# Attention of the first batch in token-tile order, with its feed-forward begun after 256 tokens

## The reference, cut to what matters

```python
scores = scale * q @ k.T + bias          # [B=4, H=8, S=576, S], masked to 0 <= i-j < 128
x = softmax(scores) @ v                  # -> [2304, 512]
x = relu(x @ w_in) ** 2 @ w_out          # 512 -> 2048 -> 512
out = sum_e P[:, e:e+1] * (relu(x @ w1[e]) @ w2[e])   # P: gate, 8 rounds of row and column scaling
```

## Time and profile before

| | |
|---|---|
| median of 3 runs | 2056.57 us (2056.37 to 2057.05) |
| the profiled execution | 2060.13 us, its span 2058.4 us |
| PE, DVE, ACT, POOL busy | 2040.2, 1292.6, 813.0, 1266.7 us |
| PE's granted clock over the span | 0.998 |
| first scores of batch 0 (L698) | 3.81 us |
| first feed-forward matmul (L737) | 51.77 us |

### The profile page before, as it was taken

How to read it: one execution, slowest core, us unless ns; L and a number is a source line. 1 busy time by engine, 2 the same in 40 slices (tenths; PEclk the granted TensorE clock), 3 DMA queues, 4 the chain that set the end, 5 groups by cost and what they waited for, 6 DMA issues and landing times.

```text
span 2058.4 us, 35904 instructions
## 1 busy us (share of the span) xinstructions
PE 2040.2 (99%) x11846; PEld 1861.4 (90%) x11846; DVE 1292.6 (63%) x2686; ACT 813.0 (39%) x1607; POOL 1266.7 (62%) x1773
## 2 busy tenths in 40 slices
PE   7999999999999999999999999999999999999999
PEld 4999999999989989989989998998998998998998
DVE  7776776756576565565575565565566555556555
ACT  6665665645333333332342332332333333333231
POOL 5333333337466666667877667667777676666663
PEclk9999999999999999999999999999999999999999
DMA  5444434322222222222232222222223222222221
GB/s 150 114 118 104 113 100 113 97 68 80 63 65 66 68 72 62 70 71 61 72 103 62 72 69 64 71 66 67 71 63 102 69 65 71 63 70 71 62 71 62
DMA packets 178081, 161.46 MB, mean 78 GB/s; under 512 B 28992, under 2 KB 127808, under 8 KB 177984
## 3 DMA queue, kind: packets, MB, share of 16 engines
q1 hardware_dynamic: 177696, 159.93, 27.6%
q10 hardware_dynamic: 288, 0.30, 0.0%
HBM read 155.47 MB, written 4.72 MB: 78 GB/s over the span
## 4 chain that ended last, share of the span: by engine, by line
PE 95%; DVE 2%; POOL 1%; ACT 1%; DMA 0%; issue 0%; DVEq 0%; ACTq 0%; SPq 0%
PE bank L854 38%; PE bank L800 34%; PE bank L744 9%; PE bank L737 9%; PE bank L728 2%; PE bank L713 2%; PE bank L702 1%; POOL xw L584 1%; DVE prob L1156 0%; POOL wl L561 0%; ACT prob L934 0%; PE bank L698 0%; PE bank L874 0%; DVE prob L1129 0%; DVE gl L1278 0%
## 5 line engine op out<-in xcount | busy, mean ns | idle before, releaser
L633 POOL TENSOR_TENSOR el<-ew,eh 128x256 fp32r<-128x256 f32 x672 | 472.4, 739 | 294.6 <-ACT eh L919 294.6
L1326 DVE SCALAR_TENSOR_TENSOR z_sb<-bank,gate,z_sb 128x512 f32<-128x512 f32 x540 | 404.0, 749 | 251.9 <-PE bank L854 251.9
L800 PE MATMUL bank<-xh,eh 128*128 128x384 f32 x1344 | 450.3, 335 | 0.0
L800 PE MATMUL bank<-xh,el 128*128 128x384 f32 x1344 | 450.2, 335 | 0.0
L854 PE MATMUL bank<-fh,gl 128*128 128x512 f32 x1152 | 450.1, 391 | 0.0
L854 PE MATMUL bank<-fl,gh 128*128 128x512 f32 x1152 | 450.0, 391 | 0.0
L800 PE MATMUL bank<-xl,eh 128*128 128x384 f32 x1344 | 449.6, 335 | 0.0
L854 PE MATMUL bank<-fh,gh 128*128 128x512 f32 x1152 | 449.1, 390 | 0.4 <-DVE z_sb L1317 0.4
L561 POOL TENSOR_TENSOR wl<-stage,wh 128x256 fp32r<-128x256 f32 x256 | 199.4, 799 | 295.2 <-ACT wh L919 294.4
L643 POOL TENSOR_TENSOR fl<-fw,fh 128x256 fp32r<-128x256 f32 x384 | 275.8, 750 | 137.3 <-ACT fh L919 136.9
L919 ACT ACTIVATE p<-bank 128x384 f32<-128x384 f32 x96 | 47.2, 492 | 668.9 <-PE bank L800 668.9
(11 more groups left out here) (112 smaller groups left out, 2924.5 us busy)
## 6 DMA issues: line engine op xcount, KB each, us to landing
fw<-in_moe_w_dram SPq DMA_DIRECT2D x96, 512.0 KB, 3.7
ew<-in_moe_w_dram SPq DMA_DIRECT2D x96, 256.0 KB, 2.8
stage<-in_moe_w_in_dram SPq DMA_DIRECT2D x64, 256.0 KB, 2.9
stage<-in_moe_w_out_dram SPq DMA_DIRECT2D x64, 256.0 KB, 2.7
a<-in_moe_w_dram SPq DMA_DIRECT2D x96, 128.0 KB, 2.7
ew<-in_moe_w_dram SPq DMA_DIRECT2D x96, 128.0 KB, 2.8
acc<-in_k_dram SPq DMA_DIRECT2D x24, 288.0 KB, 4.5
acc<-in_q_dram SPq DMA_DIRECT2D x24, 288.0 KB, 4.9
```

The source lines that it names most:

```text
L633: last = pool.tensor_tensor(el[r][:, a, :, :], ew[r][:, a, :, :], f(eh[r][:, a, :, :]), ALU.subtract)
L800: done = pe.matmul(ps, w[r][:, a, kc, :], x[:, b, kc, :], start=(first and kc == 0 and w is eh and x is xh), stop=(kc == 1 and w is el), s ...
L1326: dve.scalar_tensor_tensor(out=z, in0=ps, scalar=weight, in1=z, op0=ALU.mult, op1=ALU.add).then_inc(z_free, 1)
```

## The change

- Batch 0 takes its steps tile by tile (`place`): tile 0 of pairs 0 to 3, then tile 1 of all pairs, and so on. The tail tile has 192 keys, 64 queries (`keys_end`). The other batches keep their order.
- The stretch alone ends after ALONE = 11 slots (eight finished steps, READY, which are the first 256 tokens, and the three slots of the lag), not 22. PSUM is double-buffered only there; from slot 11 on, batch 0 has one bank for each head's scores and one for transposes.
- The feed-forward of batch 0 is cut into 256 and 320 tokens, the blocks in the order (unit 0, first), (unit 1, first), (unit 0, rest), (unit 1, rest), then units 2 and 3 as before. Slots 11 to 22 stand after groups 0, 1, 3, 4, 6, 7, 9 to 14 (`OPEN_AFTER`). The first two blocks have two result banks, and their third and fourth column blocks wait for one of these to be read.
- Weight pieces of unit 1 stand after groups 0, 1, 3, 4, 6, 7, 9, 10. Batch 1's splits begin after group 15 and its 23 slots after groups 20 to 62 (before: 3 to 60).
- At the start SP loads the first 256 columns of `kT0`, ACT (four DMAs) those of `qT0`; V of all four pairs is loaded at once, pairs 2 and 3 into an unused part of `acc` (`v_more`); then the remaining columns (eight DMAs). All pieces of unit 0 follow in the queue behind these. The two clears of `qT0` and `kT0` on DVE go.

```diff
+    FIRST = 2 * P
+    GB = max(BH, S - FIRST)
...
-        s_ps, s_odd, pT_ps = [bank[0], bank[4]], [bank[6], bank[7]], [bank[1], bank[5]]
+        s_ps, pT_ps = [bank[0], bank[4]], [bank[1], bank[5]]
+        s_odd = {1: [bank[3]], 2: [bank[6], bank[7]]}
...
+        def place(b, j):
+            return (j % KC, j // KC) if plain(b) else divmod(j, QT)
+        def keys_end(b, t):
+            return P + TAIL if plain(b) and t == FULL else 2 * P
...
+        READY = KC * (FIRST // P)
+        ALONE = READY + OUT_LAG
...
-            ev = [("v", 0), ("v", 1)]
-            for j in range(SLOTS - 1):
+            ev = []
+            for j in range(ALONE):
                 ev.append(("slot", 0, j))
-                ev += v_after(j)
-                if j % 2 and j // 2 < PIECES:
-                    ev.append(("w", j // 2))
-                if j == 4:
+                if j < PIECES:
+                    ev.append(("w", j))
+                if j == PIECES:
                     ev += [("k", 0), ("q", 0)]
...
+        OPEN_AFTER = (0, 1, 3, 4, 6, 7, 9, 10, 11, 12, 13, 14)
+        FIRST_SLOT_AFTER = (20, 22, 25, 27, 28, 30, 33, 35, 36, 38, 41, 43, 44, 46, 47, 49, 51, 52, 54, 57, 59, 60, 62)
+        FIRST_W_AFTER = (0, 1, 3, 4, 6, 7, 9, 10) + tuple(20 + k * 43 // 23 for k in range(24))
+        def block_order(w):
+            if w:
+                return [(i // 2, i % 2) for i in range(NB1)]
+            return [(0, 0), (1, 0), (0, 1), (1, 1)] + [(i // 2, i % 2) for i in range(4, NB1)]
+        def block_at(w, k):
+            edge = BH if w else FIRST
+            return (slice(0, edge), slice(edge, S))[k]
...
+            if b == 1:
+                groups.insert(6, groups.pop(8))
...
-            return 2 if b == 0 else 1
+            return 2 if plain(b) and event < ALONE else 1
...
+            early, late = slice(0, FIRST), slice(FIRST, S)
+            load_first(kT0, kf, 0, early, first_in[0])
+            load_first(kT0, kf, 1, early, first_in[1])
             sp.wait_ge(v_zero, 1)
+            load_v(0, v_sb[:, 0, :, :], v_first[0])
+            load_first(kT0, kf, 2, early, first_in[2])
+            load_first(kT0, kf, 3, early, first_in[3])
+            load_v(1, v_sb[:, 1, :, :], v_first[1])
             for i in range(2):
                 sp.dma_start(stage[:, i, :], piece1(0, i)).then_inc(w_in[i], 16)
+            for c in (2, 3):
+                load_v(c, v_more[:, c - 2, :, :], v_first[c])
+            for c in range(KC):
+                load_first(kT0, kf, c, late, rest_in[c])
+                load_first(qT0, qf, c, late, rest_in[c])
...
+                        if u == 0 and c == 0:
+                            ready = STEPS if k else READY if w == 0 else STEPS - QT + -(-BH // P)
+                            pe.wait_ge(x_lo, w * STEPS + ready)
+                        if k == 0 and c == 0:
+                            pe.wait_ge(w_split, w * (U1 * PIECES) + (u * PIECES + KC))
+                        if g == 0 and c == 0:
+                            pe.wait_ge(neg_done, ALONE)
...
+                        if anew and g and m == 0:
+                            pe.wait_ge(neg_done, (w + 1) * STEPS)
+                        for c in (((0, 1), (2, 3), (), ()) if len(ys) == 2 else ((0, 1), (2,), (3,), ()))[m]:
```

More of the change, by code:

```diff
@@ L196, in attention_moe_moe_kernel @@
         first_in = [sem(f"first_in{c}") for c in range(KC)]
-        start_in = sem("start_in")
+        rest_in = [sem(f"rest_in{c}") for c in range(KC)]
+        v_first = [sem(f"v_first{c}") for c in range(KC)]
         q_in = sem("q_in")
@@ L324, in window_events @@
             with_attention = b < B
+            if b == 1:
+                groups.insert(6, groups.pop(8))
             if with_attention:
-                for n in range(8, len(groups), 8):
+                for n in range(24 if b == 1 else 8, len(groups), 8):
                     groups[n - 1], groups[n] = groups[n], groups[n - 1]
+            for k, n in enumerate(FIRST_W_AFTER if b == 1 else W_AFTER):
+                if with_attention or k < (U1 - 1) * PIECES:
+                    after[n].append(("w", k))
             if b == 1:
[L329 to L332, removed]
+                for j in range(ALONE, SLOTS):
+                    after[OPEN_AFTER[j - ALONE]].append(("slot", 0, j))
+                after[13].append(("v", 0))
+                after[14].append(("v", 1))
+                for r in range(SPLITS):
+                    after[FIRST_SPLIT_AFTER[0][r]].append(("split", 1, 0, r))
+                after[FIRST_SPLIT_AFTER[0][2] + 1].append(("k", 1))
+                after[FIRST_SPLIT_AFTER[0][3] + 1].append(("q", 1))
             elif with_attention:
@@ L336, in window_events @@
                 for j in range(SLOTS):
-                    n = FIRST_AFTER[j] if b == 1 and j < QT else SLOT_AFTER[j]
-                    after[n] += [("slot", b, j)] + v_after(j)
+                    after[FIRST_SLOT_AFTER[j] if b == 1 else SLOT_AFTER[j]] += [("slot", b, j)] + v_after(j)
                 for c in range(1, KC + 1):
                     next_b, next_c = (b, c) if c < KC else (b + 1, 0)
-                    splits = FIRST_SPLITS[c - 1] if b == 1 and c <= 2 else SPLIT_AFTER[c - 1]
+                    splits = FIRST_SPLIT_AFTER[c] if b == 1 else SPLIT_AFTER[c - 1]
+                    loads = (splits[2] + 1, splits[3] + 1)
                     for r in range(SPLITS):
@@ L345, in window_events @@
                     if pair_number(next_b, next_c) + 1 < (B - 1) * KC:
[L346 to L347 removed]
+                        after[loads[0]].append(("k", pair_number(next_b, next_c) + 1))
+                        after[loads[1]].append(("q", pair_number(next_b, next_c) + 1))
             else:
@@ L396, in _, with load_first @@
         def _(sp):
[L397 to L405, removed]
+            def load_first(tile, src, c, at, there):
+                rows = src[2 * c:2 * c + 2, :, :].rearrange("h d s -> (h d) s")
+                sp.dma_start(tile[:, c, at], rows[:, at]).then_inc(there, 16)
             def load_twice(pair, raw, src, there):
@@ L684, in scores @@
             def scores(b, j, n):
[L685 to L689, removed]
+                c, t = place(b, j)
+                nq, k0 = span(t)
+                if plain(b) and t == 0:
                     pe.wait_ge(first_in[c], 32)
+                if plain(b) and t * P == FIRST:
+                    pe.wait_ge(rest_in[c], 32)
                 if not plain(b) and t == 0:
@@ L777, in stretch @@
-                        ys = y_banks(w)
-                        if i % 2 == 0 and m == 0:
-                            pe.wait_ge(w_split, w * (U1 * PIECES) + (i // 2 * PIECES + PIECES))
-                        for c in ((0, 1), (2,), (3,), ())[m]:
+                        u, k = block_order(w)[i]
+                        g, nt = w * NB1 + i, block_at(w, k).stop - block_at(w, k).start
+                        ys = y_banks(w, i)
+                        anew = i == 0 or len(ys) != len(y_banks(w, i - 1))
```

203 lines of the change are left out of this document (100 added, 103 removed).

## The result

The change makes the kernel slower: a median of **2066.86 us** in five runs (2064.55 to 2068.36) against 2056.57 (2056.35 to 2058.91) for the kernel before, ratio 1.0045, interval 1.0034 to 1.0057. That is +10.3 us, outside the range of the prediction and with the other sign.

A forecast was written before the change was run, and what follows sets the result against it. PE bounds the kernel from 69 us, the softmax on DVE paces the first 51.8. Gain 5.0 - 0.8 - 0.8 = 3.4 us, from the median 2056.57 to 2053.2; range 2048.7 to 2057.0, leaving out C and the best part of A.

The forecast's parts named there:

- 30.5 predicted: Start of feed-forward after the stretch alone: slot 4 at 12.2 us, then seven slots of 2.6 each; 51.8 before.
- 0.8 charged for the dense window: Batch 1's 23 slots in 43 groups instead of 58: PE stays the bound, 0.8 us lost, ends 0 and 3.
- rival C: Dense part of the window: DVE or ACT needs over 4.6 us a slot, PE waits, kernel slower; 9 in 100.
- Without any stall the same point of PE's work is reached at 30.5 + 16.3 = 46.8 instead of 51.8.: Feed-forward's start plus 16.3 us of carried scores, transposes and V products: 5.0 us saved.
- The expected gain of 5.0: Batch 0's opening: the same point of PE's work reached at 46.8 instead of 51.8 us without any stall.
- It is just covered: Slot 12: piece 8 arrives at 33 us, allowing its scores at 35.1, while PE arrives at 35.2.
- I charge 0.8 us: Twelve open slots: 0.8 us for late pieces, one bank each, and two-bank blocks waiting for DVE's copy; ends 0 and 4.
- The 4 us that I kept as the end of the range: Upper end of the stall charge over the twelve open slots: every slot losing a third.
- Rival B: Open stretch bound by DVE and ACT, normalisations slowed beside POOL, or PE at half clock; gain 0 to 1.5 us; 16 in 100.

The follow-up runs named there:

- The profile with the same order of work at clock 1.000: Batch 0's blocks cut at token 256 instead of 288, in the old order, against the kernel before: 2056.92 us against 2057.76, ratio 0.9994.
- Without piece waits: Changed kernel with unit 1's first two copies behind their slots, pieces 2 and 3 loaded earlier, batch 1's keys and queries behind group 9: 2062.19 us, 1.0021 of kernel before.

## Why the prediction was wrong

**Right.** Feed-forward started at 30.46 (30.5 predicted). The steps to it held: pair 3's slot waited for POOL's bias and began at 10.80 (11.0), as DVE's row says,

```profile
10.80 0.29 DVE L1178 CUSTOM_DVE_ANT_0 prob<-bank,bias 128x128 f32<-128x128 f32 x1 [0.42 <-POOL bias L585]
```

slot 4 at 13.15 (12.2), and six slots on from there took (28.48 - 13.15) / 6 = 2.56 each (2.6). That the sum is right to 0.1 is partly luck: slot 4 came 0.9 late, and the last step to feed-forward took 2.0 instead of 2.6. PE was through its work before slot 12 at about 35.5 (35.2). The columns of 256 and 320 cost nothing extra. From batch 1's first slot (90.10) to the 760th feed-forward matmul PE's listed waits are 1.1 (before: 0.5; 0.8 charged for the dense window), so rival C, which alone had the right sign, had the wrong place: batch 1's slots in fewer groups do little harm. The batches after are unchanged but for the 0.8 that they gain back.

**Wrong, by step.** The forecast was 3.4 faster and the medians say 10.3 slower, a miss of 13.7. Of this 9.1 is between the two profiles, 4.5 between profiles and medians.

1. *"Without any stall the same point of PE's work is reached at 30.5 + 16.3 = 46.8 instead of 51.8."* Both numbers were mis-taken. The carried work measured 17.8 for 16.3, the balance after less that before: scores 5.6, transposes 14.6 - 9.0 = 5.6, V 17.0 - 10.4 = 6.6, where I had 5.1, 5.4 and 6.2, less 0.4. (The 0.5 for the tail's scores was an estimate.) And the 51.8 belonged to an execution with the half-clock stretch of the earlier trace rows. The profile with the same order of work at clock 1.000 has 49.54, and a span 2.8 shorter. I had noted that the profiled time was 3.6 above the median and took the gain over to the median whole, but a part of what the change could win was just this stretch. The runs by clock (2057.0 at 1.000 to 2059.8 at 0.998) show that most executions had nothing there to win.
2. *The changeovers, which the sum doesn't have.* Moving twelve slots between groups adds eleven changes from V to feed-forward, nine from feed-forward to plain fp32 scores and two to the tail's transposes: 2.1 us. In the stretch alone, where PE had gaps, such a tenth of a microsecond was hidden; between groups of feed-forward it is paid. With steps 1 and 2, and without any stall, the same point of work is reached at 30.5 + 17.8 + 2.1 = 50.4 and not at 46.8. That is 1.4 before the 51.8 and 0.9 behind the 49.54. The expected gain of 5.0 was the idle time of a stretch of which the half clock, the sizes and the changeovers left most executions nothing, and every wait came on top.
3. *"It is just covered"* and *"I charge 0.8 us"*. Piece 8 came at 35.81 and not at 33. Piece 2 was 1.7 late (19.68 for 18), and while pieces 2 to 4 took 24.64 - 19.68 = 4.96 (4.95), pieces 4 to 6 took 30.82 - 24.64 = 6.2, since the load of piece 6 took 3.79 and not 2.8; why it did stays open. A cover of 0.1 us against a chain of four loads was no cover. PE waited 2.89 there, 4.5 in the twelve open slots where 0.8 was charged, and 5.7 in all; with 1.6 charged for both windows and 0.5 there before, it is 3.6 more than forecast, and some 0.9 more with the ends of the waits. The 4 us that I kept as the end of the range was the likelier value.
4. *Half clock and slowed normalisations.* Rival B had both as possibilities. The half clock came at 40.1 for 3.4 us and cost 1.4 in feed-forward's own matmuls (1.3 within the groups). The normalisations took 1.10 and 1.13 in two of the slots, 0.5 more than 0.62, near the 0.55 that rival B had; PE waited 0.8 for these two.

What the runs show as cause: the waits for pieces 3.6 us (edits taken together, and with what they do to the clock), and that what stays without them is 4.9 us. What the latter consists of comes from the balance of the traces alone. Without piece waits feed-forward began at 30.36, 19.2 before the 49.54; the carried slots take 18.2 and the changeovers 2.1, which is 1.1 more than that; the waits for DVE are 3.0 above those before, 3.8 with their ends. Together that is about the 4.9. So the larger part of it is again waits, short ones, and not the work that was moved. No run takes the changeovers or these waits away alone.

## What to carry to other kernels

Before you claim the idle time of a stretch, price the moved work at the place where it lands, changeovers included. Here the stretch with gaps hid them and the full one did not, and the gain is only the idle time less all of that. Look at whether the profiled execution is a usual one: a half-clock stretch that most executions lack is no part of what an edit can win, so compare at equal granted clock. A chain of loads in two buffers that was "just covered" on paper was 2.8 us late, and taking away its first wait alone moved it to the next piece. Short waits for the softmax follow the slots to where they are moved: charge them for each slot.

## What the runs showed of the hardware

- **Changeovers.** Into feed-forward (`128*128`) behind the product with V (`128*64`): 0.10 us more than even spacing (33 of them in the changed kernel), behind whole transposes 0.08. Out of it to the fp32 scores or the transposes of 64 rows: 0.09. To split scores and to transposes of 128 rows, both `128*128`: under 0.01.
- **A single load among others.** 256 KB landed 2.79 us after issue in the case of piece 8, 3.79 in that of piece 6 (26.88), and 5.94 behind four issues of batch 1's keys and queries.
- **Normalisation beside POOL.** Two tensor_scalar on 128x256 fp32 took 0.62 us with POOL idle and 1.10 and 1.13 while POOL made a low part.
- **The clock.** Both profiles of the kernel before have the 1.2 GHz level from 24.3 to 31.2 us, that of the same stretch alone with the cut at 256 does not. The means of the runs at 0.998 and at 1.000 are 2.8 us apart in one set (1.9 and 4.0 in two others). With PE given more to do in its gaps 11 of 12 runs had 1.000. In all five profiles with a wait of PE of 2.9 to 4.7 us behind the start of feed-forward, a stretch of 3.4 to 6.9 us at 0.50 stood at it: it began 1.1 to 1.8 us behind the wait's end in three of them (1.6 in the changed kernel), and 0.3 and 1.5 us ahead of it in two. Such a wait is not needed, though: without waits for pieces the profile has 0.50 from 30.8 to 34.2, 0.4 us behind a wait of 1.8.
